# RWKV scan and two feed-forward layers on one core: matmuls on an identity in the first slots, two staging slots, and a later lo split

## The reference, cut to what matters

```python
def _attn_ref(r, k, v, w, u):            # B 2, H 8, S 768, D 48
    state = zeros((B, H, D, D))
    for t in range(S):
        cur = einsum('bhd,bhe->bhde', u * k[t], v[t])
        y[t] = einsum('bhd,bhde->bhe', r[t], state + cur)
        state = w[t][..., None] * state + einsum('bhd,bhe->bhde', k[t], v[t])
    return y
...
xn = (x - mu) / sqrt(var + 1e-06) * g_ln               # x [2, 768, 384], g_ln [384]
x  = x + maximum(xn @ w_ch1, 0.0) @ w_ch2              # [384, 1536] and [1536, 384]
...
h = maximum(x @ w_in, 0.0)                             # [384, 1024]
u, v = h[..., :512], h[..., 512:]
v_s = einsum('ts,bsd->btd', w_spatial, normalise(v)) + b_spatial[None, :, None]
out = (u * v_s) @ w_out                                # [512, 384]
```

## Time and profile before

| | |
|---|---|
| median of 3 runs | 432.09 us (431.79 to 434.89) |
| the profiled execution's own time | 434.89 us |
| its span in the trace | 433.1 us |
| mean granted TensorE clock | 0.972 |
| PE busy | 401.7 us (93%) |
| DVE busy | 223.0 us (51%) |
| ACT busy | 147.5 us (34%) |
| POOL busy | 126.9 us (29%) |

### The profile page before, as it was taken

One profiled execution on the slowest core, in us unless ns is written; L12 is line 12 of the kernel. 1 busy time (PEld: TensorE's weight loads), 2 busy tenths in 40 slices (PEclk: granted clock), 3 DMA queues, 4 the chain that ended last, 5 costly groups with the idle time before them and its releaser, 6 DMA issues.

```text
span 433.1 us, 12371 instructions
## 1 busy us (share of the span) xinstructions
PE 401.7 (93%) x5260; PEld 373.5 (86%) x5260; DVE 223.0 (51%) x492; ACT 147.5 (34%) x328; POOL 126.9 (29%) x149
## 2 busy tenths in 40 slices
PE   2477887999999999999999899999999999999997
PEld 2465776999999999999999799999988888989897
DVE  2488879856667666657543344133236934312120
ACT  3223454353442323232324322222227712211111
POOL 3376668736442423323220431001014500000000
PEclk9998866999999999999999899999999999999999
DMA  7914324503201020110000200000060100010102
GB/s 197 330 36 130 107 91 141 166 11 121 72 24 52 21 61 10 37 60 2 3 2 3 73 2 0 2 0 2 0 219 12 62 0 0 2 54 19 38 20 91
DMA packets 26555, 24.60 MB, mean 57 GB/s; under 512 B 1666, under 2 KB 23426, under 8 KB 26500
## 3 DMA queue, kind: packets, MB, share of 16 engines
q1 hardware_dynamic: 26500, 23.80, 17.8%
HBM read 21.44 MB, written 2.36 MB: 55 GB/s over the span
## 4 chain that ended last, share of the span: by engine, by line
PE 88%; DVE 4%; issue 3%; POOL 2%; DMA 1%; ACT 1%; SPq 0%; DVEq 0%; POOLq 0%; ACTq 0%
PE bank L1200 13%; PE bank L1202 11%; PE bank L1201 11%; PE low_bank L1119 9%; PE low_bank L1200 6%; PE low_bank L1202 6%; PE low_bank L1201 6%; PE high_bank L1200 4%; PE high_bank L1201 4%; PE high_bank L1202 4%; PE bank L1167 3%; PE bank L1163 2%; PE low_bank L1083 2%; PE bank L1194 2%; DVE near L863 1%
## 5 line engine op out<-in xcount | busy, mean ns | idle before, releaser
L556 POOL TENSOR_TENSOR kin<-kin,wtot 128x256 f32<-128x256 f32 x60 | 48.8, 820 | 67.9 <-PE low_bank L1119 66.0
L1119 PEld LDWEIGHTS low_bank<-rin,kin 64*64 64x64 f32 x2048 | 39.6, 149 | 28.8 <-issue 13.7
L1119 PE MATMUL low_bank<-rin,kin 64*64 64x32 f32 x2048 | 45.1, 233 | 20.6 <-DVE near L863 8.6
L821 DVE TENSOR_TENSOR rin<-rin,wtot 128x256 f32<-128x256 f32 x60 | 36.5, 612 | 14.5 <-PE low_bank L1119 13.6
L951 DVE SCALAR_TENSOR_TENSOR h10l<-bank,h10h 128x384 fp32r<-128x384 f32 x24 | 13.4, 558 | 43.6 <-ACT h10h L695 43.6
L863 DVE COPY_PREDICATED near<-msk,low_bank 128x256 f32<-128x256 int32 x64 | 32.7, 555 | 1.4 <-PE low_bank L1083 1.4
L554 POOL TENSOR_TENSOR kin<-kin,win 128x256 f32<-128x256 f32 x12 | 12.9, 1077 | 53.1 <-PE low_bank L1119 48.9
L573 POOL TENSOR_TENSOR vrstd<-vmv,half 128x1 f32<-128x1 f32 x12 | 7.7, 644 | 70.8 <-DVE vmv L1036 70.8
L1200 PE MATMUL bank<-xnT0h,ffw 128*128 128x384 f32 x66 | 24.5, 372 | 0.0
L695 ACT ACTIVATE h11h<-bank 128x384 fp32r<-128x384 f32 x16 | 7.9, 492 | 47.7 <-PE bank L1202 47.7
L1202 PE MATMUL bank<-xnT0h,ffw 128*128 128x384 f32 x66 | 22.5, 341 | 0.0
(11 more groups left out here) (242 smaller groups left out, 1134.0 us busy)
## 6 DMA issues: line engine op xcount, KB each, us to landing
kin<-in_kT SPq DMA_DIRECT2D x12, 256.0 KB, 3.4
rin<-in_rT SPq DMA_DIRECT2D x12, 256.0 KB, 4.8
win<-in_wT SPq DMA_DIRECT2D x12, 256.0 KB, 4.3
early_stage<-in_w SPq DMA_DIRECT2D x8, 384.0 KB, 5.1
vin<-in_v SPq DMA_DIRECT2D x12, 192.0 KB, 4.0
out<-ob SPq DMA_DIRECT2D x12, 192.0 KB, 1.9
stage<-in_w SPq DMA_DIRECT2D x4, 384.0 KB, 5.6
stage<-in_w_in SPq DMA_DIRECT2D x4, 384.0 KB, 3.6
```

The source lines that it names most:

```text
L556: last = gp.tensor_tensor(k, k, wr[:, :, :, None].to_broadcast([P, NPR, m, c]), ALU.mult)
L821: last = ve.tensor_tensor(r, r, wl[:, :, :, None].to_broadcast([P, NPR, m, c]), ALU.mult)
L1119: mm = te.matmul(dst[s0:s0 + Q, NPR * e + a, :], kin[i % 4][lo:hi, a, s0:s0 + Q], r[:, :, 1, :], start=True, stop=True)
```

## The change

Three things are changed.

`keep_going` is new. In slots 0 to 19 TensorE does, behind `attend` (or behind the second level of the slot) and ahead of `gain`, `turn` and `turn_k`, three float32 matmuls of 128 by 128 on the identity, into a bank that nothing reads before it is written anew. These are 60 matmuls.

The weights go through two staging buffers alone. The hi and the lo half of a chunk now stand in the same slot (`weight_slots`), a chunk is loaded when the chunk two before it has its lo part, and the chunks of w2 are split in slots 19 to 30 instead of 16 to 29.

On VectorE, `turned_lo` now stands behind `h1_lo` and the decays of the slot, where it stood ahead of them.

```diff
+N_KEEP = 3
...
-        early_stage = place("early_stage", [P, 4, STAGE])
...
-        def hi_slots(n):
-
+        def weight_slots(n):
+
+            if n < W1C // STAGE:
+                return [1 + 3 * n, 2 + 3 * n]
             m = n - W1C // STAGE
-            return [1 + 3 * n, 2 + 3 * n] if m < 0 else [SLOT_F1 - 4 + 2 * m, SLOT_F1 - 3 + 2 * m]
-
-        def lo_slots(n):
-
-            return [k + 2 for k in hi_slots(n)]
-
-        def load_slot(n):
-
-            m = n - W1C // STAGE
-            return 3 * n - 3 if m < 0 else SLOT_F1 - 6 + 2 * m
...
+            return [SLOT_F1 - 1 + 2 * m, SLOT_F1 + 2 * m]
...
-                for n in range(2, N_FF):
-                    if load_slot(n) == k:
-                        load_chunk(n)
-            load_chunk(N_FF)
-            load_chunk(N_FF + 1)
+                for n, part in weight_parts(k):
+                    if part == 1:
+                        load_chunk(n + 2)
...
-                for n, part in weight_parts(k, lo_slots):
+                for n, part in weight_parts(k):
                     weight_lo(n, part)
...
-                if j == 3 and s >= 2:
-                    turned_lo(s - 2, "XT", (s - 2) // TG, (s - 2) % TG)
                 n = f1_of(k)
                 if n is not None:
                     h1_lo(n)
...
+                if j == 3 and s >= 2:
+                    turned_lo(s - 2, "XT", (s - 2) // TG, (s - 2) % TG)
                 if n and n % NF == 0:
                     add_f2(n // NF - 1)
...
+            def keep_going(k):
+                if k == 0:
+                    te.wait_ge(consts_loaded, 48)
+                for _ in range(N_KEEP):
+                    te.matmul(b_third[:, 0:P], idt[:, :], idt[:, :], start=True, stop=True)
...
                 n = f1_of(k)
+                if n is None:
+                    keep_going(k)
```

More of the change, by code:

```diff
@@ L186, in rwkv_moe_kernel @@
         X_SLOTS = 4
-        E_SLOTS = 4
-        slot_of = [m if m < 2 else m + X_SLOTS for m in [n % (2 + E_SLOTS) for n in range(N_FF)]] + \
-                  [n % 2 for n in range(N_FF, N_LATE)] + [2 + n for n in range(X_SLOTS)] + \
+        slot_of = [n % 2 for n in range(N_LATE)] + [2 + n for n in range(X_SLOTS)] + \
                   [n % 2 for n in range(N_ALL - N_LATE - X_SLOTS)]
         xs = x[:, :, :].rearrange("p n d -> p (n d)")
-        slots = [stage[:, q, :] for q in range(2)] + [xs[:, n * STAGE:(n + 1) * STAGE] for n in range(X_SLOTS)] + \
-                [early_stage[:, q, :] for q in range(E_SLOTS)]
+        slots = [stage[:, q, :] for q in range(2)] + [xs[:, n * STAGE:(n + 1) * STAGE] for n in range(X_SLOTS)]
         def loads_of_slot(n):
@@ L214, in rwkv_moe_kernel @@
         v_in_sbuf = [sem(f"v_in_sbuf{q}") for q in range(3)]
-        chunk_in_sbuf = [sem(f"chunk_in_sbuf{q}") for q in range(2 + X_SLOTS + E_SLOTS)]
+        chunk_in_sbuf = [sem(f"chunk_in_sbuf{q}") for q in range(2 + X_SLOTS)]
         half_set = sem("half_set")
@@ L381, in f1_of, with weight_parts @@
             return k - SLOT_F1 if k >= SLOT_F1 else None
-        def hi_slots(n):
+        def weight_slots(n):
+            if n < W1C // STAGE:
+                return [1 + 3 * n, 2 + 3 * n]
             m = n - W1C // STAGE
-            return [1 + 3 * n, 2 + 3 * n] if m < 0 else [SLOT_F1 - 4 + 2 * m, SLOT_F1 - 3 + 2 * m]
-        def lo_slots(n):
-            return [k + 2 for k in hi_slots(n)]
-        def load_slot(n):
-            m = n - W1C // STAGE
-            return 3 * n - 3 if m < 0 else SLOT_F1 - 6 + 2 * m
-        def weight_parts(k, slots_of):
+            return [SLOT_F1 - 1 + 2 * m, SLOT_F1 + 2 * m]
+        def weight_parts(k):
             for n in range(N_FF):
-                if k in slots_of(n):
-                    yield n, slots_of(n).index(k)
+                if k in weight_slots(n):
+                    yield n, weight_slots(n).index(k)
         def ff_steps():
@@ L487, in load_chunk @@
                     split_waits(sp, before[-1])
-                if 2 <= slot_of[n] < 2 + X_SLOTS:
+                if slot_of[n] >= 2:
                     sp.wait_ge(tile_turned, TR_OF_X2)
@@ L713, in _ @@
                     turned_hi(s - 2, "XT", (s - 2) // TG, (s - 2) % TG)
-                for n, part in weight_parts(k, hi_slots):
+                for n, part in weight_parts(k):
                     weight_hi(n, part)
```

## The result

The changed kernel takes 447.06 us as the median of four runs (446.99 to 450.8); the kernel before, run beside it, 431.94 (430.96 to 434.89, four runs). The ratio is 1.0359, with a 95% interval from 1.0287 to 1.0433. The forecast was 434.6 with a range up to 441: the sign leaned the right way, the size is outside.

What follows compares the result with a forecast made beforehand. It took TensorE as saturated from 76 to 230 us, and before that three engines handing each other work under an unsteady TensorE clock. -2.5 + 1.5 + 4.4 - 0.9 = +2.5 us on 432.09 gave 434.6, range 428.5 to 441.

Steps and rivals of the forecast that it cites:

- The staging: Two staging buffers, hi and lo halves in the same slot: 0.9 us gained, bounds 2 gained and 4 lost.
- halves on GpSimd lead: Rival: weight_lo waits for ScalarE and holds the next level by 0.7 us in seven slots; 439.6 us, chance 0.16.
- The 0.5 us put on a shorter gap in slot 4: TensorE's 2.82 us gap in slot 4 may shorten with one chunk less in the load queue: 0.5 us gained.
- filling without a clock: Rival: the clock still falls, so the fill costs time in slots before 20; 446.8 us, chance 0.10.
- The matmuls on the identity: Slots 0 to 19: clock stays up from slot 8, 2.5 us gained; 1.5 us lost elsewhere.
- The 2.5 us of gain: Slots 15, 11 and 19 shorten by 1.16, 0.4 and 0.9 us at a clock that stays up; bounds 0 and 5.
- the gain of 1.16: Slot 15 takes 4.04 us instead of 5.20 at the full clock, matmuls on the identity included.
- turned_lo behind h1_lo: turn_k waits for the later turned_lo in six fused slots j = 3: 4.4 us lost, bounds 0 and 7.
- The sum: All terms together: 2.5 us slower, 434.6 us, counted as no change, leaning to slower.
- SBUF and the ports: GpSimd and VectorE slow each other; no half newly beside a norm, so no change for the moved halves.

Runs made afterwards that it cites:

- e3: The changed kernel without the matmuls on the identity and with turned_lo in its old place, so the new staging alone: 450.24 us, ratio 1.0387.
- e4: The changed kernel with one edit, weight_hi_ready counted up after each half and GpSimd waiting for its own half: 435.51 us, ratio 1.008.
- e1: The kernel before plus only the three matmuls on the identity in slots 0 to 19: 432.21 us, ratio 0.9996.
- e8: The changed kernel with weight_hi_ready counted by halves and turned_lo back ahead of h1_lo: 428.96 us, ratio 0.9923.
- e11: e8 with the matmuls on the identity only in slots j = 1 and 2: 426.69 us, ratio 0.9867.
- e2: The kernel before with only turned_lo moved behind h1_lo and the decays: 438.62 us, ratio 1.0136.
- e9: e8 without the matmuls on the identity, so the staging alone with halves counted: 432.51 us, ratio 0.9999.
- e10: e8 with the matmuls on the identity left out of slots j = 3: 433.76 us, ratio 1.0012.
- e13: The kernel before plus the matmuls on the identity, halves counted, lo halves of w1 one slot behind hi, w2 halves from slot 19: 433.7 us, ratio 1.0014.

## Why the prediction was wrong, by its own steps

**The staging** is the step that failed. It said "GpSimd now waits in slots 1 and 2 for the first chunk, which is there in time", and of the w2 chunks "the engines that do it idle half of the time there ..., so nothing"; the sum had 0.9 us gained, bounds 4 lost. Measured, it is 17.9 us lost by itself (e3) and 11.5 in the whole change (e4). The reading of the rows was off in a detail: the engines that split w2 are ScalarE and GpSimd (57.23 and 58.05 us busy of 154.00), not VectorE; they idle more than half of the time. But a wait doesn't ask how busy an engine is; it asks which instruction releases it, and where that stands in its own queue. The release is a count per chunk, given one slot later, behind five copies on ScalarE (L651, L637 and L661 above) that wait for that slot's work themselves. The rival "halves on GpSimd lead" had the right engine and the right queue, "stands ahead of the next `k_left`", and 0.16; its price, 0.7 us in seven slots, was worked out from a wait for the same slot's half. The real one is 1.0 to 3.6 us in five. The first chunk, "there in time", was not: its load ends so late that the near block of slot 3 waits 0.66 us. The 0.5 us put on a shorter gap in slot 4 can't be told from the spread, 2.82 and 1.71 us in two executions of the kernel before.

The time of another rival, 446.8 for "filling without a clock", is near 447.06 by chance. Its condition was that the clock still falls in each of four slots j = 3; between 21 us and slot 20 it fell in slot 15 alone. With the wait for the second half gone (e4) it holds there too.

**The matmuls on the identity.** Their effect on the clock came as forecast: up through 41.2 to 48.0 us. Their price was a little low: six records take 0.86 us at the full clock and 1.58 at the low one (forecast 0.7 and 1.4; from start to next start in the timeline). The 2.5 us of gain was not there in e1 (0.1 us within an interval of 1.1 either way). For slot 19 I wrote "by the engine alone it would give 1.96 ...; I take 0.9": VectorE had the lead and it gave 0.0 in e1; with GpSimd out of the way it gave 1.8 (e8). For slot 15 the gain of 1.16 was eaten by the unnamed wait of 1.73 us and the clock behind it; where neither came (e11, without a fill in that slot) it takes 3.98 us. In the changed kernel the fill also softened the damage: e3, which has the staging without it, is no faster than the whole change although it has `turned_lo` early, worth 6.5 us between e4 and e8.

**turned_lo behind h1_lo.** Forecast 4.4 us in six fused slots; the waits measured are 0.61, 0.61, 1.16, 0.61, 0.56 and 0.48, 4.03 together, slot 35 the long one as said, and the slots grew by 5.2 (e2). The term missed what it does in the slots without a product: 2.0 us in e2. In the changed kernel those are 0.34 and 0.58 in slots 11 and 19.

**The sum,** by differences of medians: 447.06 less 11.5 for the halves is e4; less 6.5 for `turned_lo` (another batch) is e8 at 428.96; plus the 3.6 that the fill gained is e9 at 432.51, the time of the kernel before. Forecast were -0.9, 4.4 and -1.0. In the changed kernel the growth of 13.2 us in the fused part is 6.07 of near blocks waiting, 5.2 of the late `turned_lo` (4.03 as waits of `turn_k`; e2 and e4, which have it without the other waits, take 173.31 and 173.25 us there instead of 168.02), and at most 1.75 for 3.5 us at the low clock: 13.0 together. The 3.64 us ahead of slot 15 and its low clock ate what the fill gave before slot 20.

**SBUF and the ports.** I took GpSimd's halves as even for VectorE because none moved beside a `norm`. The trace has more such victims than `norm`: the two decays of slot 19 take 1.57 us beside halves and 0.39 without. The 1.18 us that they lose is as long as one half (1.18 to 1.22 us in e1), so the rule of the Trainium skill, page "SBUF — State Buffer", section "Who interferes with whom", that the two engines share a port pair as an exclusive lock held for the whole instruction, agrees with the row.

## What to carry to other kernels

When a step is moved closer to its producer, find the instruction that gives the count its semaphore waits for, and that instruction's place in its own engine's queue, and then who is queued behind the waiter; an idle engine is no cover for such a wait. A wait that the profile puts down to "issue" ahead of a block that used to start at once can be one of these: follow the other engines back for a few microseconds. Fill that holds TensorE's clock gave nothing in e1 and 3.6 us in e8, in part because VectorE, slowed by GpSimd, led slot 19 in e1; so it is tried again when the slots around it change. Which slots it belongs in, these runs do not settle (e8, e10, e11).

## What the runs showed of the hardware that I had not expected

- TensorE stops in the middle of a block with nothing to wait for: 1.73 us in `own_term` of slot 15 in e1 and in e8, 1.83 in slot 19 in e10, 2.67 us in slot 5 in e13, 2.82 and 1.71 us in slot 4 in two executions of the same kernel before. Every semaphore of such a block had been waited for at its first instruction. Late instructions are my guess; no run shows it.
- After the stops of 1.73 us in e1 and e8 and of 2.67 in e13, and after the waits of 3.64 and 2.33 us in the changed kernel, the granted clock is at 1.2 GHz for 3 to 7 us, though TensorE is busy again at once (56.4 to 63.2 us: busy 6.44 of 6.8). After the waits of 2.15 and 1.59 us in the fused part (slots 27 and 31) and the stop of 1.83 in e10 it stayed at 1.00. What tells the two cases apart, these runs do not show.
- Short VectorE instructions beside a GpSimd one of 1.2 us can take 1.2 us longer: two decays 0.39 us together alone (e8) and 1.57 or 1.59 beside it (e1, e13), `r_right` 0.43 and 1.23.
- The same kernel can differ from run to run by more than the changes measured here: e10's ten runs span 428.6 to 434.85 us.
